# Three attention tiles close together in each block of a fused attention, feed-forward and expert kernel

## The chip, the cores and the metric

The kernel runs on one core of one Trainium2 chip (trn2). The metric is the device time of one execution in microseconds (us); lower is better. The kernel before takes 832.36 us, the median of three runs (832.04 to 833.88).

## What is computed

Three layers on 3072 tokens (4 sequences of 768) with 512 features, all in float32.

```python
# 1. chunked attention: 8 heads of 64, chunks of 32 queries, each sees 8 memory rows
#    and its own 32 keys with 16 to the left and 8 to the right (a window of 64)
scores = scale * q_c @ k_full.T ; scores -= scores.max(-1)
a = exp(scores) ; a /= a.sum(-1) + 1e-9
x[chunk] = a @ v_full
# 2. feed-forward: 512 -> 2048 -> 512
h = x @ w_in ; g = h * cos(h) ; x = g @ w_out
# 3. one expert of 8 for each token whose skip score is positive
do_compute = x @ w_skip > 0 ; e = argmax(x @ w_gate)
out = x + gate * (relu(x @ w1[e]) @ w2[e])   # other tokens: out = x
```

## The kernel before

**Split products.** Each float32 factor of the large products is split into a high part (rounded to the matmul type) and a low part (the remainder), and three products, high*high, high*low and low*high, are summed in PSUM. ScalarE (ACT) writes the high parts, VectorE (DVE) subtracts to get the low ones.

**Blocks.** The tokens are taken in 8 blocks of 3 tiles of 128. Block B runs the feed-forward layer on its tiles in 16 steps f (`FT`): `up` (L902) makes 128 hidden columns in `h_ps` by 12 matmuls, ACT and DVE make g = h * cos(h) of them (L1167 to L1470), and two steps later `down` (L916) adds them into the three banks of `y_ps` by 9 matmuls. TensorE (PE) runs `up(f)`, `down(f-2)`, `up(f+1)` and so on without a break.

**Places between them.** Between `up` and `down`, and between `down` and the next `up`, lie numbered places, called sites in the code: site 2f stands ahead of `down`, site 2f+1 behind it. At a site a few small steps run: attention for the three tiles of block B+1, and the routing of block B-1. A tile's attention is: `scores` (PE L783, 32 small matmuls on 64x32 pieces of the array; DVE takes the maximum and subtracts), `exp` (ACT), `probs` (PE L798 turns the probabilities with 4 transposes, ACT copies them to `probsT`), `sum` (DVE), `values` (PE L821, 32 small matmuls; DVE scales into `x_sb`), `x` (PE L834, 4 transposes; ACT and DVE write the halves of `xT`, the next block's input). Routing of a tile: `x1` (PE L844, 4 transposes, DVE copies), `logits` (PE L856, 16 matmuls on 128x32 pieces), then once a block `route`, `rexp`, `gate`, `ranks` (PE L872, small) and `place`, after which GpSimd (POOL) writes the tokens' positions by an indirect DMA. The tables `ATTENTION`, `ROUTER` and `ROUTER_LAST` (L40 to L47) give the site of each step, and every engine walks the same table in order. A tile starts at site 5, 13 or 21 and uses sites +0, +1, +4, +6, +8; PE has small work at ten sites of a block (5, 9, 11, 13, 17, 19, 21, 25, 27, 29).

**Buffers.** `scores` and `values` write the same columns of `s_ps` (two PSUM banks); `probs`, `x`, `x1` and `ranks` share the bank `turn` in turns, counted by `t_full` and `t_free`. `logits` lie in another part of `s_ps`. There is one buffer each, `qk_sb` for a tile's queries and keys (768 KB) and `v_sb` for its values (512 KB).

**Loads.** All plain loads and stores go through SyncE's one queue (SP), which waits and issues strictly in the order of its program. For each tile T of a block:

```python
sp.wait_ge(s_full, T + 1)              # scores of T done: qk_sb is free
load_qk(T + 1, qk_sb[:, :, :], qk_ld)
if j == 0 and has_router(B): store(B - 1, 0..2)
sp.wait_ge(v_full, T + 1)              # values of T done: v_sb is free
load_v(T + 1, v_sb[:, :, :], v_ld)
```

On PE, `scores` of a tile waits for `qk_ld`, `values` for `v_ld`.

**Prologue and end.** Before block 0 the three tiles of block 0 run alone, in the orders `PROLOGUE_PE`, `PROLOGUE_ACT` and `PROLOGUE_DVE`, from loads of their own; filler products into `turn` (L939, L943, L950) keep PE busy. After block 7 come its routing and then 8 slots, one for each expert (`up_slot` L1074, `half` L1088), whose rows are gathered by indirect DMA into `xg` and turned by `turn_rows` (L1029). In slot 0 the rows of slot 1 are turned in the middle of `half(0, 0)`, at f = 4 of 8. `gathered_rows` (L992) brings in the first slot's early rows in two parts, one ahead of `ranks` and one behind it.

## Time and profile before

| | |
|---|---|
| median of three runs | 832.36 us (832.04 to 833.88) |
| the profiled execution | 831.3 us |
| its span, first to last instruction | 829.7 us |
| PE busy | 817.6 us (99%) |
| DVE, ACT, POOL busy | 508.5, 467.6, 75.4 us |
| moved by DMA | 93.88 MB, 113 GB/s on average |
| mean granted TensorE clock | 0.999 |

The profile comes from one execution, 1.6 us longer than its span. Busy PE includes matmuls that overlap one another, so costs of single groups are read from the chain of work that ended last, which gives each group the time until the next one could start.

### The profile page before, as it was taken

The page shows a single profiled execution, that of the slowest core. Times are in us where ns is not written, and L with a number is a line of the kernel's source. Part 1 is how long each engine was busy: PE and PEld are TensorE (multiplying, and loading weights), DVE is VectorE, ACT ScalarE, POOL GpSimd, SP SyncE. Part 2 cuts the span into 40 slices and gives each one's busy share as a digit, 9 for nine tenths or more (in the row PEclk, how much of TensorE's full clock was granted, in tenths as well). Part 3 has the DMA queues.
Part 4 walks back from the last instruction along what each step waited for, and adds up shares of the span by engine and source line. Part 5 has one row for each costly group of instructions (what it writes and reads, how often), then busy time and mean ns, then how long its engine had stood idle before and what let it go on. Part 6 is the DMA issues. An engine that isn't in the chain of part 4 may idle for free.

```text
span 829.7 us, 19685 instructions
## 1 busy us (share of the span) xinstructions
PE 817.6 (99%) x8248; PEld 724.1 (87%) x8248; DVE 508.5 (61%) x1021; ACT 467.6 (56%) x824; POOL 75.4 (9%) x96
## 2 busy tenths in 40 slices
PE   7999999999999999999999999999999999999997
PEld 5888888898888888888988898889898999999996
DVE  4678755655565556455655555565644988855563
ACT  3788665655564557655565555565545665544441
POOL 1100000010001001000100010001121342211000
PEclk9999999999999999999999999999999999999999
DMA  7952032204220421322132214202204798556300
GB/s 248 389 138 65 26 116 65 65 27 141 65 65 29 142 73 28 115 66 65 27 115 66 65 27 141 65 2 85 94 13 165 230 376 305 199 209 251 122 15 28
DMA packets 48625, 93.88 MB, mean 113 GB/s; under 512 B 9103, under 2 KB 9103, under 8 KB 48528
## 3 DMA queue, kind: packets, MB, share of 16 engines
q1 hardware_dynamic: 45040, 86.23, 30.9%
q0 software_dynamic: 3488, 6.30, 2.3%
q8 instruction: 68, 1.11, 0.6%
q14 instruction: 29, 0.24, 0.1%
HBM read 78.16 MB, written 17.00 MB: 115 GB/s over the span
## 4 chain that ended last, share of the span: by engine, by line
PE 94%; DVE 2%; issue 1%; ACT 1%; DMA 1%; POOL 0%; POOLq 0%; DVEq 0%; SPq 0%
PE y_ps L916 32%; PE h_ps L902 31%; PE h_ps L1074 10%; PE y_ps L1088 9%; PE s_ps L783 2%; PE s_ps L821 2%; PE turn L844 1%; PE turn L834 1%; PE turn L798 1%; PE s_ps L856 1%; PE turn L943 1%; DMA lists<-pairs,place 1%; PE turn L1029 0%; PE s_ps L1029 0%; DMA xg_b<-x_mid,listed 0%
## 5 line engine op out<-in xcount | busy, mean ns | idle before, releaser
L902 PE MATMUL h_ps<-xT_hi,in_hi 128*128 128x384 f32 x512 | 178.3, 348 | 0.1
L902 PE MATMUL h_ps<-xT_hi,in_lo 128*128 128x384 f32 x512 | 172.3, 337 | 0.0
L902 PE MATMUL h_ps<-xT_lo,in_hi 128*128 128x384 f32 x512 | 171.6, 335 | 0.0
L1167 ACT ACTIVATE us<-h_ps 128x384 f32<-128x384 f32 x128 | 62.4, 487 | 172.2 <-PE h_ps L902 170.3
L916 PE MATMUL y_ps<-out_hi,g_lo 128*128 128x512 f32 x384 | 151.7, 395 | 0.0
L916 PE MATMUL y_ps<-out_lo,g_hi 128*128 128x512 f32 x384 | 151.2, 394 | 0.0
L916 PE MATMUL y_ps<-out_hi,g_hi 128*128 128x512 f32 x384 | 150.7, 392 | 0.4 <-DVE g_lo L1470 0.3
L1464 DVE TENSOR_SCALAR whole<-us 128x384 f32<-128x384 f32 x128 | 47.0, 367 | 109.8 <-ACT us L1167 108.4
L902 PEld LDWEIGHTS h_ps<-xT_hi,in_hi 128*128 128x128 f32 x512 | 96.3, 188 | 3.5 <-DVE xT_lo L1364 0.3
L902 PEld LDWEIGHTS h_ps<-xT_lo,in_hi 128*128 128x128 f32 x512 | 96.4, 188 | 2.3
L902 PEld LDWEIGHTS h_ps<-xT_hi,in_lo 128*128 128x128 f32 x512 | 96.0, 188 | 0.0
L1470 DVE TENSOR_TENSOR g_lo<-hs,g_hi 128x384 fp32r<-128x384 f32 x128 | 70.8, 553 | 37.0 <-ACT g_hi L1177 37.0
L1191 ACT ACTIVATE us<-us 128x384 f32<-128x384 f32 x128 | 67.3, 526 | 41.7 <-DVE us L1466 41.4
L1459 DVE TENSOR_TENSOR hs<-hs,us 128x384 f32<-128x384 f32 x128 | 70.0, 547 | 29.3 <-ACT us L1191 25.6
L916 PEld LDWEIGHTS y_ps<-out_hi,g_lo 128*128 128x128 f32 x384 | 72.0, 188 | 15.5
L916 PEld LDWEIGHTS y_ps<-out_hi,g_hi 128*128 128x128 f32 x384 | 72.1, 188 | 14.8 <-DVE g_lo L1470 2.0
L916 PEld LDWEIGHTS y_ps<-out_lo,g_hi 128*128 128x128 f32 x384 | 72.1, 188 | 11.8
L1466 DVE TENSOR_TENSOR us<-us,whole 128x384 f32<-128x384 f32 x128 | 71.5, 559 | 4.4
L668 POOL DMA_INDIRECT lists<-pairs,place x24 | 25.2, 1048 | 524.2 <-DVE filled_to L1412 365.7
L1177 ACT ACTIVATE g_hi<-hs 128x384 fp32r<-128x384 f32 x128 | 67.0, 523 | 6.3 <-DVE hs L1459 6.3
L1074 PE MATMUL h_ps<-xgT_hi,w_hi 128*128 128x256 f32 x240 | 68.1, 284 | 0.0
L1074 PE MATMUL h_ps<-xgT_hi,w_lo 128*128 128x256 f32 x240 | 67.9, 283 | 0.0
(211 smaller groups left out, 1283.8 us busy)
## 6 DMA issues: line engine op xcount, KB each, us to landing
qk_sb<-qk SPq DMA_DIRECT2D x22, 768.0 KB, 5.2
raw_b<-w SPq DMA_DIRECT2D x32, 512.0 KB, 4.8
raw_a<-w SPq DMA_DIRECT2D x32, 512.0 KB
v_sb<-v SPq DMA_DIRECT2D x22, 512.0 KB, 3.7
x_mid<-x SPq DMA_DIRECT2D x24, 256.0 KB
out<-x SPq DMA_DIRECT2D x24, 256.0 KB
in_raw<-w_in SPq DMA_DIRECT2D x4, 1024.0 KB, 8.0
out_raw<-w_out SPq DMA_DIRECT2D x4, 1024.0 KB, 9.3
```

The costliest lines, as they stand in the source:

```text
L668: pool.indirect_dma_start(out=lists[:, :], out_offset=bass.IndirectOffsetOnAxis(ap=place[:, j:j + 1], axis=0), in_=pairs[:, j, :], in_offs ...
L902: last = pe.matmul(h_ps[:, f % 2, 0:BN], w[:, dc, f * P:(f + 1) * P], x[:, half, dc, :], start=(n == 0), stop=(n == 3 * DC - 1))
L916: last = pe.matmul(y_ps[:, j, :], g[:, f % RING, j * P:(j + 1) * P], w[:, f, :], start=(f == 0 and n == 0), stop=(f == FT - 1 and n == 2))
L1074: last = pe.matmul(h_ps[:, g % 2, (f % 2) * SLOT:(f % 2 + 1) * SLOT], w[:, dc, f * P:(f + 1) * P], x[:, dc, :], start=(n == 0), stop=(n == ...
L1088: last = pe.matmul(y_ps[:, a, :], g[:, f, a * P:(a + 1) * P], w[:, f, :], start=(f == 0 and n == 0), stop=(f == EFT - 1 and n == 2))
L1167: act.activation(us[:, f % 2, :], h_ps[:, f % 2, 0:BN], ACT.Copy, scale=1.0 / TWO_PI, bias=0.25).then_inc(us_done, 1)
L1177: act.activation(g_hi[:, f % RING, :], hs[:, f % 2, :], ACT.Copy).then_inc(ghi_done, 1)
L1191: act.activation(us[:, f % 2, :], us[:, f % 2, :], ACT.Sin, scale=TWO_PI).then_inc(cos_done, 1)
L1459: dve.tensor_tensor(hs[:, f % 2, :], hs[:, f % 2, :], us[:, f % 2, :], ALU.mult).then_inc(g_done, 1)
L1464: dve.tensor_scalar(whole[:, :], us[:, f % 2, :], ROUND, ROUND, ALU.add, ALU.subtract).then_inc(whole_done, 1)
L1466: dve.tensor_tensor(us[:, f % 2, :], us[:, f % 2, :], whole[:, :], ALU.subtract).then_inc(frac_done, 1)
L1470: dve.tensor_tensor(g_lo[:, f % RING, :], hs[:, f % 2, :], g_hi[:, f % RING, :].bitcast(F32), ALU.subtract).then_inc(glo_done, 1)
```

## The change

- **Attention in blocks 1 to 6.** Tiles start at sites 5, 9 and 13 in place of 5, 13 and 21, and a tile uses sites +0, +1, +3 (`sum`), +4 (`probs`), +8 (`values`), +12 (`x`). Three tiles meet at a site, and PE has small work at seven sites of a block: 5, 7, 9, 13, 17, 21, 25. Within a site the steps come in the order of `ORDER`, `values` first and `scores` after `x` and `probs`. Block 0 keeps its sites.
- **Routing.** `x1` of all tiles and all `logits` come at sites 5, 7 and 9, `route` at 10, `ranks` at 21.
- **PSUM.** `values` moves to columns 256 to 511 of both banks of `s_ps`, `x` to columns 0 to 255 of both, `x1` of tile 1 to `s_ps` too. `x1T` has two buffers, the shared turn counters become one pair for each kind of step.
- **Loads.** The host's layout of queries, keys and values is one row of 6 KB and 4 KB for each partition; a tile's queries and keys come by two DMAs (256 and 512 KB) in place of one, with rows of 2 and 4 KB. SP's order of waits and loads is untouched.
- **Prologue.** The 64 short filler products go, of two long ones behind the first `scores` one is left and is a quarter shorter. `x` of tile 1 comes ahead of `values` of tile 2 (with a buffer `x_pre`), `sum` of tile 2 ahead of `values` of tile 0 on DVE.
- **End.** `turn_rows(1)` comes at f = 6 in place of f = 4, and three of the four parts of `gathered_rows` come ahead of `ranks`, in place of two.

```diff
-ATTENTION = []
-for _j, _b in enumerate((5, 13, 21)):
-    ATTENTION += [(_b, "scores", _j), (_b + 1, "exp", _j), (_b + 4, "probs", _j), (_b + 4, "sum", _j),
-                  (_b + 6, "values", _j), (_b + 8, "x", _j)]
-ROUTER = [(5, "x1", 0), (9, "logits", 0), (11, "x1", 1), (13, "logits", 1), (19, "x1", 2), (21, "logits", 2),
-          (24, "route", 0), (25, "rexp", 0), (26, "gate", 0), (27, "ranks", 0), (28, "place", 0)]
-ROUTER_LAST = [(5, "x1", 0), (6, "logits", 0), (7, "x1", 1), (8, "logits", 1), (9, "x1", 2), (10, "logits", 2),
-               (10, "route", 0), (11, "rexp", 0), (12, "gate", 0), (12, "ranks", 0), (13, "place", 0)]
+ORDER = ("values", "x", "probs", "scores", "exp", "sum")
+
+
+def attention(first, period, probs, values, x):
+
+    sites = {}
+    for j in range(3):
+        b = first + j * period
+        for site, step in ((b, "scores"), (b + 1, "exp"), (b + 3, "sum"), (b + probs, "probs"), (b + values, "values"),
+                           (b + x, "x")):
+            sites.setdefault(site, []).append((step, j))
+    return {site: sorted(steps, key=lambda x: ORDER.index(x[0])) for site, steps in sites.items()}
+
+
+FIRST_ATTENTION = attention(5, 8, 4, 6, 8)
+ATTENTION = attention(5, 4, 4, 8, 12)
+ROUTER = {5: [("x1", 0), ("x1", 1)], 7: [("logits", 0), ("logits", 1), ("x1", 2)], 9: [("logits", 2)], 10: [("route", 0)],
+          11: [("rexp", 0)], 12: [("gate", 0)], 21: [("ranks", 0)], 22: [("place", 0)]}
+ROUTER_LAST = {5: [("x1", 0), ("x1", 1)], 7: [("logits", 0), ("logits", 1), ("x1", 2)], 9: [("logits", 2)], 10: [("route", 0)],
+               11: [("rexp", 0)], 12: [("gate", 0)], 13: [("ranks", 0)], 14: [("place", 0)]}
...
 PROLOGUE_PE = [("scores", 0), ("scores", 1), ("probs", 0), ("scores", 2), ("probs", 1), ("values", 0), ("probs", 2),
-               ("values", 1), ("x", 0), ("values", 2), ("x", 1), ("x", 2)]
-PROLOGUE_ACT = [("exp", 0), ("probs", 0), ("exp", 1), ("probs", 1), ("exp", 2), ("probs", 2), ("w_in", 0), ("x", 0), ("w_in", 1),
-                ("x", 1), ("x", 2), ("w_in", 2)]
-PROLOGUE_DVE = [("scores", 0), ("scores", 1), ("sum", 0), ("scores", 2), ("sum", 1), ("values", 0), ("sum", 2),
-                ("values", 1), ("x", 0), ("values", 2), ("x", 1), ("x", 2)]
+               ("values", 1), ("x", 0), ("x", 1), ("values", 2), ("x", 2)]
+PROLOGUE_ACT = [("exp", 0), ("probs", 0), ("exp", 1), ("probs", 1), ("exp", 2), ("probs", 2), ("w_in", 0), ("x", 0),
+                ("x", 1), ("w_in", 1), ("x", 2), ("w_in", 2)]
+PROLOGUE_DVE = [("scores", 0), ("scores", 1), ("sum", 0), ("scores", 2), ("sum", 1), ("sum", 2), ("values", 0),
+                ("values", 1), ("x", 0), ("x", 1), ("values", 2), ("x", 2)]
...
+def steps_of(B, last):
+
+    tables = [{} if B == 0 else ROUTER_LAST if B == last else ROUTER,
+              FIRST_ATTENTION if B == 0 else {} if B == last else ATTENTION]
+    return {site: [x for table in tables for x in table.get(site, [])] for site in sorted(set().union(*tables))}
...
-        x1T = sb("x1T", [P, DC, P])
+        x1T = sb("x1T", [P, 2, DC, P])
...
-        qk_sb = sb("qk_sb", [P, 3, 512])
-        v_sb = sb("v_sb", [P, 2, 512])
+        q_sb = sb("q_sb", [P, HP, P])
+        k_sb = sb("k_sb", [P, HP, CPT, WIN])
+        v_sb = sb("v_sb", [P, CPT, HP * HD])
...
-        qk_pre = pre("qk_pre", [P, 2, 3, 512])
-        v_pre = pre("v_pre", [P, 2, 2, 512])
+        q_pre = pre("q_pre", [P, 2, HP, P])
+        k_pre = pre("k_pre", [P, 2, HP, CPT, WIN])
+        v_pre = pre("v_pre", [P, 2, CPT, HP * HD])
...
+        x_pre = pre("x_pre", [P, HP, 2, HD])
...
-            return y_ps[:, 1:3, 0:HP * HD] if is_first(B) and j != 1 else s_ps[:, :, 0:HP * HD]
+            return y_ps[:, 1:3, 0:HP * HD] if is_first(B) and j != 1 else s_ps[:, :, 256:512]
...
         def x_bank(B, j):
-            return (h_ps[:, 0, :], h_ps[:, 1, :], s_ps[:, 0, :])[j] if is_first(B) else turn[:, 0, :]
...
+                return pieces((h_ps[:, 0, :], h_ps[:, 1, :], s_ps[:, 0, :])[j])
+            return pieces(turn[:, 0, :] if B == 0 else s_ps[:, :, 0:256])
+
+        def rows_of(xT, half, j):
+            return xT[:, 1 - half, :, j * P:(j + 1) * P].rearrange("p (a c) n -> p a c n", a=2)
+
+        def x1_bank(j):
+            return pieces(s_ps[:, :, 256:512] if j == 1 else turn[:, 0, :])
...
-            def load_qk(tile, to, ld):
-                sp.dma_start(to, qk[tile, :, :, :].rearrange("r p n -> p r n")).then_inc(ld, 16)
-
-            def load_v(tile, to, ld):
-                sp.dma_start(to, v[tile, :, :, :].rearrange("r p n -> p r n")).then_inc(ld, 16)
+            def load_qk(tile, to_q, to_k, ld):
+                sp.dma_start(to_q, qk[bass.ds(tile, 1), :, 0:HP * P].rearrange("a p n -> (a p) n")).then_inc(ld, 16)
+                sp.dma_start(to_k, qk[bass.ds(tile, 1), :, HP * P:].rearrange("a p n -> (a p) n")).then_inc(ld, 16)
+
+            def load_v(tile, to_v, ld):
+                sp.dma_start(to_v, v[bass.ds(tile, 1), :, :].rearrange("a p n -> (a p) n")).then_inc(ld, 16)
...
-                            load_qk(T + 1, qk_sb[:, :, :], qk_ld)
+                            load_qk(T + 1, flat(q_sb), flat(k_sb), qk_ld)
...
                             sp.wait_ge(v_full, T + 1)
-                            load_v(T + 1, v_sb[:, :, :], v_ld)
...
-                        pe.wait_ge(qk_ld, 16 * loads_of(B, j))
+                        pe.wait_ge(qk_ld, 32 * loads_of(B, j))
...
-                        pe.wait_ge(v_free, T)
+                        if B == 0 or j == 0:
+                            pe.wait_ge(v_free, T)
+                        if B > 0 and j == 0:
+                            pe.wait_ge(x_free, T)
...
+                        wait(pe, p_free, j - 1)
+                    elif B == 0:
+                        pe.wait_ge(x_free, T)
+                    elif j == 0:
+                        pe.wait_ge(x1_free, BT * B)
                     else:
-                        turn_is_free(B, step, j)
+                        pe.wait_ge(p_free, T)
...
+                    elif B == 0:
+                        pe.wait_ge(s_free, T + 1)
+                    elif j == 0:
+                        pe.wait_ge(s_free, T + 2)
+                        pe.wait_ge(route_step, ROUTE * (B - 1) + CHOSEN + 1)
+                    elif j == 1:
+                        pe.wait_ge(s_free, T + 2)
+                        pe.wait_ge(v_free, T)
                     else:
-                        pe.wait_ge(s_free, T + 1)
+                        pe.wait_ge(v_free, T)
+                        pe.wait_ge(x_free, T - 1)
...
+                    elif B == 0:
+                        pe.wait_ge(p_free, T + 1)
+                    elif j == 0:
+                        pe.wait_ge(s_free, T + 3)
                     else:
-                        turn_is_free(B, step, j)
+                        pe.wait_ge(x_free, T)
                     pe.wait_ge(v_free, T + 1)
...
+                    if j == 0 and B > 1:
+                        pe.wait_ge(ranks_free, R)
+                    elif j == 2:
+                        pe.wait_ge(x1_free, BT * R + 1)
+                    else:
+                        pe.wait_ge(x_free, BT * (B + 1))
+                        pe.wait_ge(v_free, BT * (B + 1))
...
+                    pe.wait_ge(x1_free, BT * R + max(j + 1, 2))
+                    if j == 0 and not is_last(B):
+                        pe.wait_ge(s_free, BT * (B + 1) + 1)
...
-                    turn_is_free(B, step, j)
+                    if is_last(B):
+                        pe.wait_ge(x1_free, BT * B)
+                    else:
+                        pe.wait_ge(p_free, BT * (B + 2))
...
-            for n in range(64):
-                c = slice((n % 4) * 32, (n % 4 + 1) * 32)
-                pe.matmul(turn[c, 0, 0:NL], ident[:, c], ident[:, 0:NL], start=True, stop=True)
-            def long_products(n):
+            def long_products(n, columns=4):
 
                 for _ in range(n):
-                    pe.matmul(turn[:, 0, :], ident[:, :], ident[:, :].unsqueeze(1).to_broadcast([P, 4, P]), start=True, stop=True)
+                    pe.matmul(turn[:, 0, 0:columns * P], ident[:, :], ident[:, :].unsqueeze(1).to_broadcast([P, columns, P]),
+                              start=True, stop=True)
...
-                    long_products(2)
+                    long_products(1, 3)
                 elif (step, j) == ("probs", 0):
                     long_products(1)
-                elif (step, j) == ("x", 1):
+                elif (step, j) == ("values", BT - 1):
                     keep_running(turn[:, 0, 0:P], 3)
...
-            gathered_rows(0)
+            gathered_rows((0, 1, 2))
             pe.wait_ge(route_step, ROUTE * (BLOCKS - 1) + CHOSEN)
             ranks().then_inc(last_ranks_full, 1)
-            gathered_rows(1)
+            gathered_rows((3,))
...
-                    if s == 0 and a == 0 and f == EFT // 2:
+                    if s == 0 and a == 0 and f == EFT - 2:
                         turn_rows(1)
...
-                    wait_probs_turned(act, B, j)
+                    act.wait_ge(p_full, T + 1)
                     wait(act, v_full, T - 1 if is_first(B) else T)
                     act.activation(turned_probs(B, j)[:, :, :].rearrange("p h q -> p (h q)"), probs_bank(B, j),
-                                   ACT.Copy).then_inc(first_free if is_first(B) else t_free, 1)
+                                   ACT.Copy).then_inc(p_free, 1)
                 elif step == "x":
-                    wait_x_turned(act, B, j)
+                    act.wait_ge(x_full, T + 1)
+                    if B > 0 and j < BT - 1:
+                        act.wait_ge(v_free, T + 2)
...
+                    if not is_first(B):
+                        wait(dve, v_free, T - 1)
...
-                    if not (is_first(B) and j == 0):
-                        wait_x_turned(dve, *((B, j - 1) if j else (B - 1, BT - 1)))
-                    dve.tensor_tensor(x_sb[:, :, :, :].rearrange("p h a d -> p a h d"),
+                    if not is_first(B):
+                        dve.wait_ge(x_full, T)
+                    elif j == 2:
+                        dve.wait_ge(x_full, 1)
+                    if B > 0 and j == 0:
+                        dve.wait_ge(s_full, T + 3)
...
-                    dve.wait_ge(t_full, use(B, step, j) + 1)
-                    wait(dve, lg_full, BT * (B - 1) + j)
-                    dve.tensor_copy(x1T[:, :, :].rearrange("p c n -> p (c n)"), turn[:, 0, :]).then_inc(t_free, 1)
+                    dve.wait_ge(x1_full, BT * (B - 1) + j + 1)
+                    if j == 1 and not is_last(B):
+                        dve.wait_ge(s_full, BT * (B + 1) + 1)
+                    wait(dve, lg_full, BT * (B - 1) + max(0, j - 1))
+                    dve.tensor_copy(x1T[:, j % 2, :, :].rearrange("p (a c) n -> p a c n", a=2), x1_bank(j)).then_inc(x1_free, 1)
```

Its order on SP, for one block (1 to 6). Before, the loads around the first tiles (`qk_sb` queries and keys, `v_sb` values, `x_mid` and `out` the routed block's stores):

```order
L473 DMA qk_sb<-qk 128x3x512 [waits s_full]
L492 DMA x_mid<-x_60 128x512 [waits y_free]
L493 DMA out<-x_60 128x512
L492 DMA x_mid<-x_60 128x512 [waits y_free]
L493 DMA out<-x_60 128x512
L492 DMA x_mid<-x_60 128x512 [waits y_free]
L493 DMA out<-x_60 128x512
L476 DMA v_sb<-v 128x2x512 [waits v_full]
L473 DMA qk_sb<-qk 128x3x512 [waits s_full]
L476 DMA v_sb<-v 128x2x512 [waits v_full]
```

The same stretch of SP's program after the change:

```order
L451 DMA q_sb<-qk 128x512 [waits s_full]
L452 DMA k_sb<-qk 128x1024
L471 DMA x_mid<-x_60 128x512 [waits y_free]
L472 DMA out<-x_60 128x512
L471 DMA x_mid<-x_60 128x512 [waits y_free]
L472 DMA out<-x_60 128x512
L471 DMA x_mid<-x_60 128x512 [waits y_free]
L472 DMA out<-x_60 128x512
L455 DMA v_sb<-v 128x1024 [waits v_full]
L451 DMA q_sb<-qk 128x512 [waits s_full]
L452 DMA k_sb<-qk 128x1024
L455 DMA v_sb<-v 128x1024 [waits v_full]
```

The order of kinds on SP did not move; the load of queries and keys became two instructions.

PE at site 21 before, where `scores` of the third tile stands (`x1T` and `wr` are the routing operands, L902 the next `up`):

```order
L856 MATMUL s_ps<-wr,x1T 32x9 [waits t_free]
L856 MATMUL s_ps<-wr,x1T 32x9 x15
L783 MATMUL s_ps<-qk_sb 32x64 [waits v_free,qk_ld,s_free]
L783 MATMUL s_ps<-qk_sb 32x64 x31
L834 MATMUL turn<-ident,x_sb 128x128 [waits v_free,t_free]
L834 MATMUL turn<-ident,x_sb 128x128 x3
L902 MATMUL h_ps<-xT_hi,in_hi 128x384 [waits h_free]
```

PE at site 13 after the change, where `scores` of the third tile stands now (L813 is `values` of the first tile, L781 `probs` of the second, L762 `scores` of the third, L904 the next `up`):

```order
L813 MATMUL s_ps<-v_sb,probsT 32x64 [waits route_step,s_free,p_free,v_ld]
L813 MATMUL s_ps<-v_sb,probsT 32x64 x31
L781 MATMUL turn<-ident,probs 128x128 [waits exp_done,p_free]
L781 MATMUL turn<-ident,probs 128x128 x3
L762 MATMUL s_ps<-k_sb,q_sb 32x64 [waits qk_ld,s_free]
L762 MATMUL s_ps<-k_sb,q_sb 32x64 x31
L904 MATMUL h_ps<-xT_hi,in_hi 128x384 [waits h_free]
```

`scores` of the third tile moved from site 21, two sites behind `values` of the second tile, to the end of the site that begins with `values` of the first.

## Rows read from the trace of the kernel before

**Rows 1.** The page, its head: span, and busy time of each engine.
```profile
span 829.7 us, 19685 instructions
...
PE 817.6 (99%) x8248; PEld 724.1 (87%) x8248; DVE 508.5 (61%) x1021; ACT 467.6 (56%) x824; POOL 75.4 (9%) x96
```

**Rows 2.** Chain of waits, 230 to 320 us: start us, us, what.
```profile
242.91 0.79 PE s_ps L821 x53
243.70 2.28 PE h_ps L902 x12
...
266.61 2.09 PE h_ps L902 x12
...
274.98 0.37 PE s_ps L856 x32
...
280.11 0.79 PE s_ps L821 x53
280.90 0.59 PE turn L844 x4
...
293.70 2.07 PE y_ps L916 x9
295.77 0.44 PE turn L798 x4
```

**Rows 3.** Timeline of SP's queue, 264 to 345 us: start us, us, issue.
```profile
280.93 0.38 SPq L476 DMA_DIRECT2D v_sb<-v  x1
```

**Rows 4.** Tile qk_sb, then v_sb, 70 to 560 us (18 loads each).
```profile
DMA to landing us min/median/max: 4.5/5.2/7.0
...
DMA to landing us min/median/max: 3.4/3.7/4.4
```

**Rows 5.** Stretches: PE, PEld, DVE, ACT, POOL busy, clock, DMA share, GB/s.
```profile
4.00:6.00 2.00, 2.00 (x3) 0.70 (x3) 0.00 (x0) 0.00 (x0) 0.00 (x0) 1.00 1.02 381
```

**Rows 6.** Timeline of DVE, 262 to 346 us: the last step ahead of a `down`.
```profile
292.81 0.56 DVE L1470 TENSOR_TENSOR g_lo<-hs,g_hi 128x384 fp32r<-128x384 f32 x1 [1.79 <-ACT g_hi L1177]
```

**Rows 7.** Chain of waits, 0 to 33 us.
```profile
1.71 1.89 PE turn L939 x128
3.60 3.71 PE turn L943 x4
...
8.30 1.91 PE turn L943 x4
...
14.08 2.26 issue
```

**Rows 8.** DMA issues of 1 to 5 us: KB each, median us to landing.
```profile
in_raw<-w_in SPq DMA_DIRECT2D x1, 1024.0 KB, 13.3
```

**Rows 9.** Timelines of SP, DVE, ACT and PE, 0 to 40 us.
```profile
4.60 0.90 SPq L481 DMA_DIRECT2D in_raw<-w_in  x1
...
23.26 0.62 ACT L1129 ACTIVATE in_hi<-in_raw 128x512 fp32r<-128x512 f32 x1
...
24.14 0.44 PE L902 MATMUL h_ps<-xT_hi,in_hi 128*128 128x384 f32 x1
```

**Rows 10.** Timeline of PE, 636 to 667 us, idle before in brackets.
```profile
641.39 1.16 PE L992 MATMUL s_ps<-ident,xg_a 128*128 128x128 f32 x8
642.83 0.18 PE L872 MATMUL turn<-chosen,preceding 128*128 128x8 bf16 x1 [0.29 <-DVE chosen L1432]
...
661.58 0.39 PE L1088 MATMUL y_ps<-w_hi,eg_lo 128*128 128x512 f32 x1
662.80 0.66 PE L1029 MATMUL turn<-ident,xg_b 128*128 128x128 f32 x4 [0.82 <-DMA xg_b<-x_mid,listed]
```

**Rows 11.** PE's last product, and the stretches after it (columns of rows 5).
```profile
823.72 0.39 PE L1088 MATMUL y_ps<-w_hi,eg_lo 128*128 128x512 f32 x1
...
824.00:826.00 2.00, 0.10 (x1) 0.00 (x0) 0.75 (x1) 0.00 (x0) 0.11 (x1) 1.00 0.05 12
826.00:828.00 2.00, 0.00 (x0) 0.00 (x0) 0.00 (x0) 0.00 (x0) 0.86 (x1) 0.80 0.30 111
```

170 lines of the change are left out of this document (61 added, 109 removed).

## The prediction

> **What bounds the kernel now.** I read the page's head first: PE is busy for 817.6 of 829.7 us [rows 1]. No other engine comes near, so the time changes by what PE executes and by what it is made to wait for. The next view is the chain of waits in a middle block [rows 2]. It is PE from end to end. The two large groups, 12 matmuls of `up` and 9 of `down`, take 2.09 and 2.07 us, and between them lie the small groups at their own prices: `scores` or `values` 0.79, four transposes 0.44, `logits` 0.37. One more price is to be seen there. A group that follows one with 32-column pieces (L783, L821, L856) takes longer: transposes 0.59 in place of 0.44, `up` 2.28 in place of 2.09. So each excursion to small pieces costs PE 0.15 to 0.19 us on top. Third, SP's queue and the landings [rows 3, 4], since two buffers with one load in flight each sit behind `scores` and `values`. PE shows no wait for them now.
>
> **Fewer sites, the same groups.** A block has the same 9 sets of transposes, 3 `scores`, 3 `values`, 3 `logits` and `ranks` as before. What differs is how often small pieces are entered. Before there are 7 excursions a block (sites 5, 9, 11, 13, 19, 21, 27). After there are 8: one each at 5, 7, 17 and 21, two at 9 (`logits`, transposes, `scores`) and two at 13 (`values`, transposes, `scores`). Sites as such cost nothing: transposes alone at a site cost the same 0.44 as behind others [rows 2]. That makes +0.17 us a block, +1.0 over six blocks. In block 7 `logits` of two tiles come together, one excursion fewer, -0.1. Sum: **+0.9 us**. Entering small pieces straight from transposes is not in this chain. Its bounds are no surcharge of its own, and another 0.17 us at the three such points of a block, +3.1 in all; I take none, since the excursion is already charged once.
>
> **DVE and ACT.** They get the same instructions, closer together. The margin to watch is `g_lo`, ready at 292.81 + 0.56 = 293.37 for a `down` that starts at 293.70 [rows 2, 6]: 0.33 us, behind a site with `scores`, whose exponential sits in ACT's queue. Site 13 now has `values` ahead of `scores` on DVE, but the exponential waits for h anyway. I add nothing; what covers it is that margin.
>
> **The third tile's load.** This is the large term. SP waits in its program's order, and that order is the old one: after the stores it waits for `values` of tile 0, loads `v` of tile 1, and only then may load queries and keys of tile 2, though their buffer came free with `scores` of tile 1. Before, `values` of tile 0 stood at site 11 and `scores` of tile 2 at site 21, so this cost nothing. Now both stand at site 13, with only one set of transposes between them. So `scores` of tile 2 waits for a transfer that is issued when `values` of tile 0 ends. Step by step from that end:
> - `values` ends at 280.11 + 0.79 = 280.90 and SP issues at 280.93 [rows 2, 3]: 0.03 us.
> - 512 KB of `v` go first in the same queue and land after 3.7 us, median of 18 [rows 4].
> - 768 KB of queries and keys follow. At the 381 GB/s of back-to-back loads [rows 5] they need 2.06 us more, so they are there at 5.79 us.
> - PE has 0.44 us of transposes meanwhile. It stands for **5.35 us**.
>
> This happens in blocks 1 to 6, in block 0 not, whose sites are kept: 6 x 5.35 = **+32.1 us**. Bounds: if `v` cost the transfer behind it nothing, 5.2 us for one load of queries and keys [rows 4], so 4.8 us of wait and +28.7; if the landings simply added, 3.7 + 5.2 = 8.9, so 8.5 and +51. The truth is near the lower one, as the second load's start-up runs beside the first one's data. The other two tiles are covered: the load for `scores` of tile 1 is issued at site 5, two pairs of `up` and `down` (8.4 us) ahead of site 9, and the longest landing with stores behind it is 7.0 us [rows 4]. `v` has 8.4 us each time. While PE stands, DVE stands too (its `values` waits for that `scores`), so nothing is gained back behind the wait.
>
> **The clock after each stand.** After PE's last product (823.72 + 0.39 = 824.11) the granted clock averages 0.80 in 826 to 828: full for 1.2 us, then half, so it fell at 827.2, 3.1 us after the work stopped [rows 11]. A stand of 5.35 us can therefore let it fall to 1.2 GHz. At the start, PE ran at half speed from 1.71 to at least 7.31 us: four records took 3.71 us, later the same four 1.91 [rows 7]. So a fall costs up to half of about 6 us, 3.0 us, and at least some of it, say 1. The stand at 14.08 of 2.26 us did not bring it down. I take a fall in four stands of six, at 2.0 us each: **+8 us**; bounds 0 and +18. The Trainium skill, page TensorE: Matmul & The Clock Gate, section HAM oscillation, says that a wait for a DMA between bursts of products can put the clock back to half and that every burst then starts cold. By that rule the term would be +18 in place of +8; what hangs on it is the second rival.
>
> **Prologue.** The 64 filler products (1.89 us) and one long product go, but loads bound what follows. The first piece of `w_in` lands at 4.60 + 13.3 = 17.9 us [rows 8, 9], and ACT's order keeps its conversion ahead of `x`. Behind it stand eight steps of the shape 128x512 (its conversion, `x` of tile 0 high and low, tile 1 low, `values` and transposes of tile 2, high and low), at 0.62 each [rows 9] 5.0 us: block 0 starts at 22.9 in place of 24.14. **-1.2 us.** Bounds: 0, if a break like the 2.26 us in `values` of tile 0 [rows 7], where no semaphore is waited for, lands worse in the shorter program, and -2.3 if it goes and its whole length counts.
>
> **End.** A product of 512 columns is followed by the next after 2.07 / 9 = 0.23 us, so PE stood from 661.58 + 0.23 = 661.81 to 662.80, 0.99 us, ahead of `turn_rows(1)` [rows 2, 10]. The two steps f moved ahead of it, 6 products or 1.4 us, cover that. Late next is the split of those rows by ACT and DVE, about 2 x 0.6 us, and the two last steps f, again 1.4 us, cover it with little to spare. Against it, the third part of `gathered_rows` takes a quarter of two times 1.16 us, 0.58, where PE had 0.29 us free ahead of `ranks`, and others wait for `ranks`: +0.2. **-0.8 us.**
>
> **Sum.** 831.3 + 0.9 + 32.1 + 8 - 1.2 - 0.8 = 870.3 us for an execution like the profiled one, which lies 1.1 us under the median of the runs; so **871 us**.
>
> **The rivals.**
> - *The clock falls in every stand*, for its whole 3.0 us: 870.3 - 8 + 18 + 1.1 = 881 us. For it: 5.35 us is well over the 3.1 us of [rows 11]. Against it: the moment of the fall need not fit each stand.
> - *It never falls*: 863 us. For it: the 2.26 us stand left no trace. Against it: the fall after 3.1 us at the end.
> - *Other side: the third tile's load arrives unseen.* If queries and keys were there within 0.44 us of the end of `values`, through a semaphore already high enough or a load issued at site 9, the change would do what it says, and 832.4 + 0.9 - 1.2 - 0.8 = 831.3 us come out, not slower. Against it: both orders in the section on the change leave SP no way around its wait for `values`, and the wait of `scores` counts both of its own DMAs.
> - *DVE falls behind at the fuller sites.* Past the margin of 0.33 us `down` waits for `g_lo`; with one transposing step's 0.6 us more on DVE at two sites a block that would be 12 x 0.3 to 12 x 0.6, 4 to 7 us on top, 877 us.
>
> **How the numbers follow.** Forecast 0.36; clock falls always 0.26; never 0.30; DVE behind 0.05; other side 0.03. The range takes in the low bound of the wait with the never-falling clock and a good prologue, 831.3 + 0.9 + 28.7 - 2.3 - 0.8 + 1.1 = 859, and reaches on the other end past 881 by some of the wait's upper bound: 857 to 885. A measurement of this kernel can tell about 0.2%, 1.7 us, from no change. The other side's 831.3 is 0.13% under the median, so its chance goes mostly to the middle: faster 0.01, same 0.02, slower 0.97.
>
> **What would show it.** In the changed kernel's PE timeline, each of blocks 1 to 6 has one idle stretch of some 5 us right ahead of the third tile's `scores`, released by the load into `k_sb`, and none elsewhere; SP issues `v`, `q` and `k` in one row just behind `values`; the landing from SP's issue of `v` is near 5.8 us. PE's busy time stays near 817 us if the clock holds, and the clock line shows dips where it does not. The first `up` starts near 22.9 us. The prediction is wrong if these stretches are missing, or if they are there and shorter than 4.8 us. It is wrong in the sum of small terms if the six blocks, less their waits, do not come out within 0.5 us of the blocks before.

## The result, and the profile after

The changed kernel takes 879.38 us, the median of four runs (878.89 to 881.08), where the kernel before takes 832.2 us in the same session (four runs, 831.29 to 833.88). The ratio is 1.056, with a 95% interval of 1.0545 to 1.058: 47 us slower. The forecast was 871 us with a range of 857 to 885.

The head of the page after, beside [rows 1]:

```profile
span 877.3 us, 19437 instructions
...
PE 828.1 (94%) x8118; PEld 735.7 (84%) x8118; DVE 511.6 (58%) x1021; ACT 468.8 (53%) x824; POOL 75.5 (9%) x96
...
PEclk8999998999899989998999999899999999999999
```

PE's share falls from 99% to 94%: some 50 us in which it does nothing, where there were 12. Its busy time grows by 10.5 us although it executes 130 matmuls fewer, so part of the work ran slower. The clock line, all nines before, now has dips in the middle of the blocks. The waits of PE in the changed kernel (engine, line, tile, releaser: us in total, times, longest):

```profile
PE s_ps L762 <- DMA k_sb<-qk: 34.1, 7, 6.0
PE y_ps L918 <- DVE g_lo L1474: 3.3, 4, 1.0
...
PE h_ps L1074 <- DVE eg_lo L1593: 0.8, 1, 0.8
PE turn L1029 <- DMA xg_b<-x_mid,listed: 0.8, 1, 0.8
```

The first line is the forecast stall. One of its seven, 0.2 us, is in the prologue; in the blocks there are six, 33.9 us in all, 5.65 us each. The second line had 0.3 us and one entry before; three more of 1.0 us each are new and were not forecast. PE's timeline around the stall of block 2 (start us, us, engine, line, operation; idle before it and what released it):

```profile
219.01 0.86 PE L813 MATMUL s_ps<-v_sb,probsT 64*32 64x64 f32 x64
219.80 0.66 PE L781 MATMUL turn<-ident,probs 128*128 128x128 f32 x4
226.22 1.17 PE L762 MATMUL s_ps<-k_sb,q_sb 64*32 64x64 f32 x64 [5.77 <-DMA k_sb<-qk]
227.33 0.69 PE L904 MATMUL h_ps<-xT_hi,in_hi 128*128 128x384 f32 x1
227.81 0.52 PE L904 MATMUL h_ps<-xT_lo,in_hi 128*128 128x384 f32 x1
...
230.15 0.34 PE L904 MATMUL h_ps<-xT_hi,in_hi 128*128 128x384 f32 x1
230.33 0.34 PE L904 MATMUL h_ps<-xT_lo,in_hi 128*128 128x384 f32 x1
```

And SP's queue in the same stretch, to be held against [rows 3]:

```profile
219.90 0.33 SPq L455 DMA_DIRECT2D v_sb<-v  x1
220.27 0.43 SPq L451 DMA_DIRECT2D q_sb<-qk  x1
220.75 0.43 SPq L452 DMA_DIRECT2D k_sb<-qk  x1
```

`values` (L813) gives way to the transposes at 219.80, SP issues `v` at 219.90 and `q` and `k` in one row behind it. PE has 0.66 us of transposes (0.44 where other work follows them at once; here the last one runs out) and then stands until 226.22, 6.32 us after SP's first issue. The chain of events is the forecast one. The `up` products that follow (L904) come 0.32 us apart, from 230.15 on 0.18 us: the first 3.7 us after the stall run at half the clock. The granted clock in short stretches (PE, PEld, DVE, ACT, POOL busy, clock, DMA share, GB/s):

```profile
220.00:222.00 2.00, 0.46 (x4) 0.21 (x2) 1.83 (x7) 1.92 (x3) 0.00 (x0) 1.00 0.46 162
222.00:224.00 2.00, 0.00 (x0) 0.00 (x0) 0.68 (x2) 1.01 (x2) 0.00 (x0) 0.77 0.98 332
...
226.00:228.00 2.00, 1.78 (x66) 1.64 (x67) 0.47 (x1) 0.00 (x0) 0.00 (x0) 0.50 0.04 8
228.00:230.00 2.00, 2.00 (x9) 2.00 (x8) 1.84 (x5) 0.00 (x0) 0.00 (x0) 0.53 0.00 0
230.00:232.00 2.00, 2.00 (x11) 1.78 (x10) 0.90 (x3) 1.09 (x3) 0.00 (x0) 1.00 0.00 0
```

A mean of 0.77 in 222 to 224 is full speed for 1.08 us and then half, so the clock fell from 2.4 to 1.2 GHz at 223.1, 2.6 us after the last transposes ended (219.80 + 0.66 = 220.46). It was back at 229.9. The same sum over the other five stalls gives 6.83 us at half speed in each, of which 3.4 to 4.3 us, mean 3.8, lie behind the restart. All six stalls let it fall. (The dip at the line's beginning is one more fall, in the prologue: half speed from 14.9 to 21.7 us.)

Where the time went, from the two timelines. "Blocks" is the time from the first `up` of block 0 to the first product behind the last `down` of block 7:

| profiled execution | first `up` | blocks | from there to the end | span |
|---|---|---|---|---|
| before | 24.14 | 614.6 | 191.0 | 829.7 |
| after | 23.08 | 662.3 | 191.9 | 877.3 |
| difference | -1.1 | +47.7 | +0.9 | +47.6 |

### The profile page after: what moved, and what is told of

Same layout as the page of the kernel before. It is cut to its first block and busy times, and to the rows that moved or that the text cites. A ratio compares the mean times of both kernels' runs of the same rounds, so it can differ in the third digit from the quotient of the medians.

```text
span 877.3 us, 19437 instructions
## 1 busy us (share of the span) xinstructions
PE 828.1 (94%) x8118; PEld 735.7 (84%) x8118; DVE 511.6 (58%) x1021; ACT 468.8 (53%) x824; POOL 75.5 (9%) x96
## 5 line engine op out<-in xcount | busy, mean ns | idle before, releaser
L904 PE MATMUL h_ps<-xT_hi,in_hi 128*128 128x384 f32 x512 | 181.2, 354 | 0.0
L904 PE MATMUL h_ps<-xT_hi,in_lo 128*128 128x384 f32 x512 | 175.0, 342 | 0.0
L904 PE MATMUL h_ps<-xT_lo,in_hi 128*128 128x384 f32 x512 | 174.9, 342 | 0.0
L904 PEld LDWEIGHTS h_ps<-xT_hi,in_hi 128*128 128x128 f32 x512 | 98.8, 193 | 6.0 <-issue 1.0
L904 PEld LDWEIGHTS h_ps<-xT_lo,in_hi 128*128 128x128 f32 x512 | 98.9, 193 | 3.0
L904 PEld LDWEIGHTS h_ps<-xT_hi,in_lo 128*128 128x128 f32 x512 | 98.4, 192 | 0.0
L1463 DVE TENSOR_TENSOR hs<-hs,us 128x384 f32<-128x384 f32 x128 | 71.0, 555 | 28.3 <-ACT us L1192 21.7
L1074 PE MATMUL h_ps<-xgT_lo,w_hi 128*128 128x256 f32 x240 | 68.0, 283 | 0.0
```

The source lines that it names most:

```text
L904: last = pe.matmul(h_ps[:, f % 2, 0:BN], w[:, dc, f * P:(f + 1) * P], x[:, half, dc, :], start=(n == 0), stop=(n == 3 * DC - 1))
L1074: last = pe.matmul(h_ps[:, g % 2, (f % 2) * SLOT:(f % 2 + 1) * SLOT], w[:, dc, f * P:(f + 1) * P], x[:, dc, :], start=(n == 0), stop=(n == ...
L1463: dve.tensor_tensor(hs[:, f % 2, :], hs[:, f % 2, :], us[:, f % 2, :], ALU.mult).then_inc(g_done, 1)
```

## The experiments

Eight kernels, in two groups of four, each group with its own runs of the kernel before (832.93 and 832.94 us). Two questions stood: whether the stall and the clock are the whole of the loss, and what the small terms are, which the forecast had put at zero or near it.

My theory: the third tile's load is issued too late by SP's order, and each stall also costs half speed behind it; the block-0 waits come from `sum` on DVE. The main rival: the fuller places are dear in themselves.

### e1_order: SP's loads in the order of the places

```diff
-                    for j in range(BT):
-                        T = tile_of(B, j)
-                        following = not (isinstance(T, int) and T == NT - 1)
-                        if following:
+                    todo = ["qk0", "store", "v0", "qk1", "v1", "qk2", "v2"] if B == 0 else \
+                           ["qk0", "store", "qk1", "v0", "qk2", "v1", "v2"]
+                    for what in todo:
...
```

> The changed kernel with SyncE's loads in the order in which the places now give their buffers back: in the blocks from 1 on, queries and keys of the third tile (whose scores are in front of the values of the second) are issued ahead of those values' wait. No transfer is added or removed. My theory (the third tile's load is issued only behind the values of the second and stops TensorE 5.65 us in each of six blocks, and each stop brings one fall of the clock that costs about 1.5 us): the row 's_ps <- qk' of 34.1 us goes to under 1, the granted clock is back near 0.99, and the time is 879.4 - 34 - 9 = 836 us, 833 to 839. Rival A, the places themselves are dearer (fuller sites, DVE behind): the wait goes but the block stays over 80 us, 850 or more. Rival B, the load is late through its landing and not through its issue: the stall only shrinks and the time is 860 to 875.

(What the text above calls the values of the second tile is `values` of the block's first tile, tile 0 in the prediction's count; what SP loads behind that wait is the second tile's `v`.)

**Measured:** 835.41 us, median of 10 (833.48 to 835.95), ratio to before 1.002 (1.0005 to 1.0035). Of the 47 us, 44 are gone with an order of issues. PE's waits:

```profile
PE y_ps L923 <- DVE g_lo L1479: 3.4, 4, 1.0
...
PE h_ps L767 <- DMA k_pre<-qk: 1.1, 1, 1.1
```

No wait for `k_sb` is left in the blocks, and the granted clock between 100 and 600 us is 1.00, where the changed kernel has 0.96. The blocks take 618.8 us: 43.5 less than in the changed kernel. 33.9 of them are the stalls, so 9.6, or 1.6 us for each stall, is the half speed. Rivals A and B fall: fuller places alone would have left 850 us, a slow landing 860.

### e2_order_sum: and `sum` of block 0 where it was

```diff
-FIRST_ATTENTION = attention(5, 8, 4, 6, 8)
+FIRST_ATTENTION = attention(5, 8, 4, 6, 8, 4)
```

(the sixth number is the distance of `sum`, 3 in the changed kernel and 4 before).

> The kernel e1_order with one more edit: in block 0 the sum stands four sites behind the scores, as before the change, instead of three. My theory (in block 0 `down` waits 1.0 us at three places for g_lo, since VectorE does the sum ahead of the fraction): the waits of down for g_lo there go from 3.3 us to under 0.5 and the time is 3.0 us under e1_order, about 833. Rival (TensorE loses that time at the next place in some other way, or the waits come from the prologue's order): the time is within 1 us of e1_order.

**Measured:** 831.63 us, median of 10 (829.93 to 832.66), ratio to before 0.9973 (0.9959 to 0.9987). That is 3.8 us under e1_order in the medians; in the traces the blocks are 3.1 us shorter, 615.7, and PE's waits for `g_lo` are down from 3.4 to 0.3 us. DVE's timeline in the changed kernel shows the cause:

```profile
42.34 0.55 DVE L1463 TENSOR_TENSOR hs<-hs,us 128x384 f32<-128x384 f32 x1
42.81 0.68 DVE L1347 TENSOR_REDUCE row_sum<-probs 128x8 f32<-128x512 f32 x1
43.53 0.17 DVE L1349 TENSOR_SCALAR row_sum<-row_sum 128x8 f32<-128x8 f32 x1
43.73 0.20 DVE L1351 RECIPROCAL row_sum<-row_sum 128x8 f32<-128x8 f32 x1
43.85 0.31 DVE L1468 TENSOR_SCALAR whole<-us 128x384 f32<-128x384 f32 x1
44.20 0.56 DVE L1470 TENSOR_TENSOR us<-us,whole 128x384 f32<-128x384 f32 x1
44.67 0.55 DVE L1474 TENSOR_TENSOR g_lo<-hs,g_hi 128x384 fp32r<-128x384 f32 x1
```

The three steps of `sum` take 1.04 us (42.81 to 43.85) right between two steps of g = h * cos(h), and the `down` that needs `g_lo` starts 1.0 us late:

```profile
45.28 0.50 PE L918 MATMUL y_ps<-out_hi,g_hi 128*128 128x512 f32 x1 [0.99 <-DVE g_lo L1474]
```

With `sum` one site later the same three steps stand behind `g_lo` and cost nothing. The middle blocks show no such wait in the changed kernel although `sum` stands at +3 there too. What e2_order_sum leaves against the kernel before is 615.7 - 614.6 = +1.1 us in the blocks, the price of the seven places themselves. It is a small difference between single traces, but the four traces that share this block program (e2_order_sum, e6_turn4, e7_short, e8_ranks) lie within 0.2 us of each other.

### e3_swap: the stall kept, `v` taken out of the third tile's way

```diff
-                        if following:
+                        if following and not (B > 0 and j == 1):
                             sp.wait_ge(s_full, T + 1)
...
                             sp.wait_ge(v_full, T + 1)
+                            if B > 0 and j == 0:
+                                sp.wait_ge(s_full, T + 2)
+                                load_qk(T + 2, flat(q_sb), flat(k_sb), qk_ld)
                             load_v(T + 1, flat(v_sb), v_ld)
```

> The changed kernel with the wait kept and only two issues exchanged: in the blocks from 1 on SyncE still waits for the values of the second tile, and then issues queries and keys of the third ahead of the load of the second's values. My theory (the stall is issue plus the landing of v and then of q and k one behind the other): q and k land without v's bytes in front, so the stall of 5.65 us becomes 5.65 - 1.3 (the piece of 256 KB at 200 GB/s, or 0.7 at the 381 GB/s of the sum) = 4.3 to 5.0, six times; the clock still falls in each block; the time is 879.4 - 4 to 8 = 871 to 875. Rival (the landing is latency, not bytes): the stall stays at 5.3 or more and the time at 877 or more.

**Measured:** 871.2 us, one run. The wait shrank as forecast:

```profile
PE s_ps L765 <- DMA k_sb<-qk: 26.4, 6, 5.8
```

26.4 / 6 = 4.40 us in place of 5.65: the 512 KB of `v` ahead cost the load of `q` and `k` 1.25 us on the mean. (The expectation spoke of a piece of 256 KB at 200 GB/s; what stood ahead is `v`, 512 KB, which at the 381 GB/s of [rows 5] would be 1.4 us.) The single stalls run from 3.62 to 5.78 us, and SP's queue tells part of why. An issue takes it 0.3 to 0.5 us, but some take 1.2 us or more; the first stall has this one:

```profile
134.67 1.89 SPq L452 DMA_DIRECT2D k_sb<-qk  x1
```

The two stalls with such a long issue are the two longest here, 5.24 and 5.78 us; in the changed kernel two have one as well. Without them it is 3.86 us here (four stalls) against 5.54 (four), so `v` ahead costs 1.7 us like for like. The landing is start-up and bytes together, not latency alone. The blocks became 6.2 us shorter though the stalls became 7.5 shorter. The clock shows why:

```profile
222.00:224.00 2.00, 0.00 (x0) 0.00 (x0) 0.57 (x2) 1.01 (x2) 0.00 (x0) 0.88 1.02 370
224.00:226.00 2.00, 1.68 (x66) 1.54 (x67) 0.37 (x1) 0.00 (x0) 0.00 (x0) 0.50 0.33 131
226.00:228.00 2.00, 2.00 (x8) 2.00 (x7) 1.84 (x5) 0.00 (x0) 0.00 (x0) 0.50 0.00 0
228.00:230.00 2.00, 2.00 (x8) 1.90 (x7) 0.44 (x1) 0.33 (x1) 0.00 (x0) 0.50 0.00 0
230.00:232.00 2.00, 2.00 (x10) 1.59 (x9) 0.92 (x2) 1.97 (x4) 0.00 (x0) 0.92 0.00 0
```

Work restarts at 224.32 and runs at half speed until 230.3, 6.0 us, where in the changed kernel it was 3.7. In this block the shorter stall did not end the slow stretch earlier, so more of that stretch met work. Over the six stalls 25.8 us of work lie at half speed here, 22.9 in the changed kernel, although two of the slow stretches were only half as long.

### e4_fill: the stall filled with products that nobody reads

```diff
+                    if B > 0 and j == 2:
+                        pe.wait_ge(s_free, T)
+                        for _ in range(20):
+                            pe.matmul(s_ps[:, 0, 0:P], ident[:, :], ident[:, :], start=True, stop=True)
                     if ahead:
                         pe.wait_ge(pre_qk_ld[j - 1], 32)
```

> The changed kernel with 20 products of 128 columns ahead of the third scores in the blocks from 1 on, into PSUM columns that are free and are written again: TensorE works where it stood still, and still waits for the rest. 20 products take some 5 us at half speed or 1.5 to 2.5 at full, less than the stall of 5.65, so they add nothing to the wait. My theory (a stop brings the clock down about 3 us after the work ends, and the half speed then costs 1.5 us of the following work in each of six blocks): the pause that is left is about 3 us, the clock falls in few blocks or in none, and the time is 879.4 - 6 to 9 = 870 to 873 with a granted clock above 0.98. Rival (the half speed lies beside the stall and costs nothing): the clock rises and the time stays within 1 us of 879.4. Other rival (the pause that is left still brings the clock down, later): clock and time stay.

**Measured:** 867.85 us, one run; the blocks take 653.5 us, 8.8 less than in the changed kernel. PE still stands 1.3 us on the mean behind the fillers:

```profile
PE s_ps L766 <- DMA k_sb<-qk: 7.6, 6, 2.2
```

and the clock never falls in the blocks; the same stretch as above and the whole of 100 to 600 us:

```profile
222.00:224.00 2.00, 0.97 (x9) 0.78 (x7) 0.00 (x0) 0.00 (x0) 0.00 (x0) 1.00 0.74 287
224.00:226.00 2.00, 0.85 (x65) 0.79 (x65) 0.00 (x0) 0.00 (x0) 0.00 (x0) 1.00 0.03 10
...
100.00:600.00 500.00, 492.35 (x5390) 439.75 (x5389) 274.85 (x621) 273.93 (x506) 22.10 (x30) 1.00 0.19 65
```

This prices the clock alone: 8.8 us, 1.5 for each stall. The transfers came no earlier: from the end of `values` to the third tile's `scores` it is 6.4 us on the mean here and 6.3 in the changed kernel. The rival by which half speed lay beside the stall and cost nothing falls. Two parts of the expectation were missed. The 20 products took 4.6 us at full speed and not 1.5 to 2.5, so that 0.4 to 2.2 us of the pause were left and not some 3; and the time is 2 us under the range of 870 to 873. For that the clock is not the reason: of the 11.1 us between the two spans (877.3 and 866.2) some 2.4 lie outside the blocks. Block 0 starts 0.5 us earlier, and the part behind the blocks is 1.9 us shorter, for the reason told under e6_turn4.

### e5_adjacent: each place enters small pieces once

```diff
+ATTENTION[9] = [("probs", 0), ("logits", 2), ("scores", 1)]
+ATTENTION[13] = [("probs", 1), ("values", 0), ("scores", 2)]
...
+    if tables[0] is ROUTER and tables[1] is ATTENTION:
+        tables[0] = {site: steps for site, steps in ROUTER.items() if site != 9}
```

> The kernel e2_order_sum (831.6) with two places of blocks 1 to 6 in another order: at 9 probs, logits, scores in place of logits, probs, scores, and at 13 probs, values, scores in place of values, probs, scores. The same groups of products, but small pieces are entered once at each of these places and not twice. My price of an excursion (0.15 to 0.19 us each, charged in the prediction as +0.9 for one more a block): 2 x 0.17 x 6 = 2.0 us less, 829.6, and the six blocks come out 1.0 us under those of before. Rival, an excursion between small groups costs nothing and the +1.1 of the places has another source: 831.6 within 0.5. Other rival, values at 13 now waits for nothing but ACT's copy comes later and down waits for g_lo: over 832.

**Measured:** 829.91 us, median of 11 (827.13 to 830.45), ratio to before 0.9955 (0.9941 to 0.9969). The forecast was 829.6. The blocks take 613.1 us, 2.6 less than in e2_order_sum and 1.5 less than before. Place 13 in PE's timeline, first e2_order_sum:

```profile
286.20 0.86 PE L818 MATMUL s_ps<-v_sb,probsT 64*32 64x64 f32 x64
286.99 0.66 PE L786 MATMUL turn<-ident,probs 128*128 128x128 f32 x4
287.58 0.86 PE L767 MATMUL s_ps<-k_sb,q_sb 64*32 64x64 f32 x64
288.37 0.44 PE L909 MATMUL h_ps<-xT_hi,in_hi 128*128 128x384 f32 x1
```

then e5_adjacent:

```profile
284.85 0.60 PE L790 MATMUL turn<-ident,probs 128*128 128x128 f32 x4
285.38 0.86 PE L822 MATMUL s_ps<-v_sb,probsT 64*32 64x64 f32 x64
286.04 0.85 PE L771 MATMUL s_ps<-k_sb,q_sb 64*32 64x64 f32 x64
286.82 0.44 PE L913 MATMUL h_ps<-xT_hi,in_hi 128*128 128x384 f32 x1
```

From the start of the last `down` product (285.88 and 284.62) to the start of `up` it is 2.49 us in the first and 2.20 in the second, for the same three groups: 0.29 us saved at this place. At place 9 it is 0.15 (2.07 and 1.92), the same in all six blocks, and six times both sums is the 2.6 us. An excursion to small pieces has a price of its own, and this is the fastest kernel of the study, faster than both the kernel before and the changed one.

### e6_turn4: `turn_rows(1)` back at f = 4

```diff
-                    if s == 0 and a == 0 and f == EFT - 2:
+                    if s == 0 and a == 0 and f == EFT // 2:
```

> The kernel e2_order_sum with turn_rows(1) back at f = 4 of half(0, 0), as before the change. My theory (moving it covers PE's stand for the gathered rows by two steps f, 1.4 us; the end did not become shorter in the changed kernel's profile only because the lists landed 1.0 us later in that execution): the stand ahead of turn_rows is 0.8 us if the lists land as early as before, or 1.8 to 2.2 if late, and the time is 0.8 to 1.4 us over e2_order_sum, 832.4 to 833.0. Rival (what the later turn saves is given back by up_slot(1, 0), which waits 0.8 to 1.0 us for eg_lo): the time is within 0.3 us of 831.6.

**Measured:** 832.63 us, median of 10 (831.21 to 833.97), 1.0 over e2_order_sum. The two were timed in different groups, and their intervals against before overlap (0.9979 to 1.0007 here), so the traces have to speak. The part behind the blocks depends on when `listed`, the read-back of the tokens' positions, lands. GpSimd waits for it ahead of the gather. In the changed kernel (first row; second row the PE stand for the gathered rows):

```profile
706.61 1.27 POOL L660 DMA_INDIRECT xg_b<-x_mid,listed  x1 [8.00 <-DMA listed<-lists]
...
710.73 0.66 PE L1029 MATMUL turn<-ident,xg_b 128*128 128x128 f32 x4 [0.76 <-DMA xg_b<-x_mid,listed]
```

Before, the same wait was 6.96 us. Over all the traces it is near 7.0 or clearly longer:

| `turn_rows(1)` at | POOL's wait for `listed` | part behind the blocks |
|---|---|---|
| f = 4 | 7.0 (before, e6_turn4) | 191.0, 191.0 |
| f = 6 | 7.0 to 7.1 (e3_swap, e4_fill, e7_short, e8_ranks) | 190.2, 190.0, 190.3, 190.7 |
| f = 6 | 7.6 to 8.3 (after, e1_order, e2_order_sum, e5_adjacent) | 191.9, 192.1, 192.0, 191.7 |

With the early landing the later turn saves 0.6 us on the mean, and no stand for the gathered rows over 0.2 us is left (e6_turn4 has one of 1.04 us, where 0.8 was expected); with the late landing the part is 1.6 us longer. The traces show two ways of being late. GpSimd waits for the first of eight reads that SP issues in a row. In e1_order SP issues it 18.1 us behind the blocks, in all others at 17.4 to 17.6, and GpSimd goes on 2.8 us after the issue, as in the early ones. In the other three late ones it goes on 3.8 to 4.0 us after it, and there the second or third issue of the row holds SP for 1.2 to 1.9 us in place of 0.47; in the early ones none of the first five does. The rival has its grain: `up_slot(1, 0)` waits 0.6 to 1.0 us for `eg_lo` in the four late ones, and this is within the 1.6, and 0.4 in e8_ranks; e6_turn4 has none of it.

### e7_short: the 64 short fillers back

```diff
+            for n in range(64):
+                c = slice((n % 4) * 32, (n % 4 + 1) * 32)
+                pe.matmul(turn[c, 0, 0:NL], ident[:, c], ident[:, 0:NL], start=True, stop=True)
             def long_products(n, columns=4):
```

> The kernel e2_order_sum with the 64 short filler products back ahead of the first scores. My theory (the prologue is bound by the loads, and they lay beside them): block 0 starts at 22.8 us within 0.2, the time is 831.6 within 0.5. Rival A (they keep the clock up through the prologue): block 0 starts 0.5 or more earlier, 831. Rival B (PE is what bounds the prologue's head and they cost their 1.9 us): block 0 starts at 24 or later, 833 or more.

**Measured:** 832.34 us, median of 10 (830.52 to 834.84), 0.7 over e2_order_sum. PE's timeline at the start:

```profile
1.70 1.90 PE L946 MATMUL turn<-ident 128*32 128x9 f32 x128 [1.70 <-POOL ident L610]
3.53 3.16 PE L950 MATMUL turn<-ident 128*128 128x512 f32 x4
6.62 0.86 PE L767 MATMUL s_ps<-k_sb,q_sb 64*32 64x64 f32 x64
...
23.79 0.44 PE L909 MATMUL h_ps<-xT_hi,in_hi 128*128 128x384 f32 x1
```

and in e2_order_sum:

```profile
1.70 3.78 PE L947 MATMUL turn<-ident 128*128 128x512 f32 x4 [1.70 <-POOL ident L610]
5.41 1.06 PE L767 MATMUL s_ps<-k_sb,q_sb 64*32 64x64 f32 x64
...
22.77 0.45 PE L909 MATMUL h_ps<-xT_hi,in_hi 128*128 128x384 f32 x1
```

The first `scores` starts 1.2 us later with them, and block 0 1.0 us later. I expected no effect; this is between my theory and rival B. The fillers were in the way of the first tile. One caution: the start of block 0 varies by itself. Over the kernels with one and the same prologue it lies at 22.53 to 23.23 us in seven traces, and at 24.92 in that of e8_ranks, where PE waits 2.2 us for `k_pre` in place of 0.3 to 1.4. The clock has a part in this: in e2_order_sum, e4_fill and e5_adjacent it did not fall in the prologue, and block 0 starts at 22.77, 22.60 and 22.53; in e1_order, e3_swap and e6_turn4 it was at half speed for 3.4 us there, and block 0 starts at 22.96, 23.23 and 23.14. The trace of e7_short has such a fall of 3.4 us too, so its 23.79 is to be held against the latter three: 0.7 us.

### e8_ranks: the parts of `gathered_rows` as before

```diff
-            gathered_rows((0, 1, 2))
+            gathered_rows((0, 1))
...
-            gathered_rows((3,))
+            gathered_rows((2, 3))
```

> The kernel e2_order_sum with two of the four parts of gathered_rows ahead of ranks and two behind, as before the change. The prediction charged the move of one part +0.2 us, since PE had only 0.29 us free ahead of ranks and the part takes 0.58. My theory now (PE stands 0.33 us for hot a little later, so the order within this stretch is free): the time is 831.6 within 0.3 and the stretch from the last down to the lists' DMA is unchanged at 9.5 us. Rival (the charge was right): 0.2 less, the lists' DMA is issued 0.2 us earlier.

**Measured:** 831.75 us, median of 10 (830.13 to 832.92), 0.1 over e2_order_sum. In both, GpSimd issues the first write of the lists 9.5 us behind the blocks. PE waits 0.29 us for `chosen` ahead of `ranks` here, and 0.33 us for `hot` a little later there: the wait only changes its place. The charge of 0.2 us is within what these medians can't tell, so the run shows no effect and does not exclude it.

## Why the forecast was right, and where its steps were off

The forecast of a slower kernel, its mechanism and its place held; the time came out 8 us over the forecast, inside the range. Every term of the sum came out somewhat over its forecast, and inside the clock's term two errors nearly cancel. By the terms of its sum, for the profiled execution (870.3 forecast, 878.9 measured):

| term | forecast | measured | from |
|---|---|---|---|
| the third tile's wait | +32.1 | +33.9 | changed kernel's waits |
| half clock behind it | +8 | +9.6 (8.8 by e4_fill) | e1_order |
| fewer places | +0.9 | +1.1 | e2_order_sum |
| `sum` ahead of g in block 0 | 0 | +3.1 | e1_order less e2_order_sum |
| prologue | -1.2 | -1.1 | first `up` |
| end | -0.8 | +0.9 | part behind the blocks |

- **The wait.** 5.35 us was worked out as 0.03 + 3.7 + 2.06 - 0.44. It took 5.65 on the mean. Term by term, means of the six: SP's issue 0.10, `v` landed after 3.59, `q` and `k` 2.48 behind it, PE started 0.14 later, less 0.66 of transposes. The term that was short is the third: 768 KB behind 512 took 2.5 us and not 2.06, so the 381 GB/s of [rows 5] were too fast for them (two of the six have one of SP's long issues). Both bounds (4.8 and 8.5) held it, and the choice near the lower one was right.
- **The clock.** Right in its total, by two errors that nearly cancel. I took four falls of six at 2.0 us; there were six at 1.6. The rival with a fall in every stand had the count right and the price wrong. It took half of 6 us; in fact 3.8 us of the 6.83 at half speed met work, 1.1 of them `scores`, which took 1.11 us in place of 0.79. By the rule of the Trainium skill, page TensorE: Matmul & The Clock Gate, section HAM oscillation, which was weighed there, a wait for a DMA between bursts can put the clock back to half and each burst then starts cold. All six stalls of the trace, 5.0 to 6.0 us, agree with it; the six waits of 0.4 to 2.2 us in e4_fill did not start cold. The prediction calls the rival that hangs on the rule the second; it is the first of its list. Its +18 us was too high, since 3.0 of the 6.83 us at half speed had passed while PE still stood, and the 1.1 us of `scores` lost only 0.3.
- **The places.** The price of an excursion, 0.17 us, is confirmed from both sides, a little low: over blocks 1 to 6 one more a block gave +1.2 us where +1.0 was forecast (468.8 in e2_order_sum, 467.6 before), and two fewer a block (e5_adjacent) -2.6 where -2.0 was. So the nearest value is 0.20 to 0.22 us.
- **DVE behind.** This was the step that failed: "I add nothing; what covers it is that margin". I looked at site 13 of the middle blocks and at the margin of 0.33 us, and both held: the middle blocks have no wait for `g_lo`. But `sum` had moved from +4 to +3 in all blocks, block 0 included, whose sites I had taken as kept, in the section on the change too. The fixed `b + 3` in the new table says otherwise. 1.04 us of DVE work ahead of g against a small margin gives the 1.0 us stand, three times.
- **Prologue.** The sum was right, its reason only in part. I let the conversion of `w_in` and ACT's order set the start and gave the fillers no weight; e7_short puts some 0.7 us on the fillers, so most of the 1.1 us comes from the first `scores` starting earlier. The break in `values` was 0.7 us shorter in the profiled execution (1.54 for 2.26), but the clock was at half speed for 6.8 us of its prologue, so the agreement is in part luck.
- **End.** The -0.8 is nearly right like for like (0.6 less at the same landing), but the profiled execution had the late landing of `listed`, 1.6 us. The +0.2 for the moved part of `gathered_rows` has no support: e8_ranks shows no effect.
- **The other side.** 831.3 us was the price of the change without the stall. With the load's order and the `sum` mended, e2_order_sum gives 831.6.
- **The signs.** The stalls were where they were said to be, and none was shorter than 4.8 us. But "none elsewhere" failed by the three stands in block 0, and the last sign came true: blocks 1 to 6 less their waits are 478.6 us against 467.6, and even without the slow clock (468.8 in e2_order_sum) they miss the 0.5 us. The sign was badly set, as the forecast's own +1.0 lies outside it.

Left open: what decides whether SP's long issues fall on the read of `listed` or on a load that PE waits for, and the spread of the prologue's loads. Neither was tried.

## What to carry to other kernels

When steps move closer together, move the queue's waits with them: a loader that walks "all of tile 0, then all of tile 1" is only right while the compute walks so too. Here 44 of the 47 us lost were one line of order. With that mended the new schedule was still 0.2% slower than the old; with `sum` put back as well it was 0.3% faster, and with its small pieces put together 0.45%. Read every distance in a schedule's table, for the special first round as well; a step that moves by one place can pass from behind a critical chain to inside it. Of a stall as long as these (4 to 6 us), charge also the slow clock behind it, and charge only the part of the slow stretch that meets work; where the stall can't be removed, work that fills it was worth 1.5 us each time here.
